# The opening of a fused attention and two-expert-layer kernel: first loads, first mask, sink loads, order of transposes and evacuations

## The reference

```python
# q, k, v: (2, 8, 768, 64); n_sink = 4, window = 128
scores = scale * np.matmul(q, k.transpose(0, 1, 3, 2))
keep = is_sink | in_window                  # key < 4, or 0 <= query - key < 128
scores = np.where(keep, scores, -1e9)
a = softmax(scores)
x = (a @ v) as (1536, 512)                  # heads side by side

h = x @ w_in                                # (512, 2048)
y = (max(h, 0) + alpha * min(h, 0)) @ w_out # (2048, 512)

e = argmax(y @ w_gate)                      # 8 experts, 384 places each
out = gate * (max(y @ w1[e], 0) @ w2[e])    # (512, 1024), (1024, 512)
```

## Time and profile before

| | us |
|---|---|
| median of 3 runs | 615.85 |
| lowest and highest | 614.84, 617.77 |
| the profiled execution | 616.75 |
| its span in the profile | 615.0 |
| PE busy in the span | 594.3 |
| PE's first matmul of scores | 6.5 |
| first matmul of `hidden(0)` | 41.18 |

### The profile page before, as it was taken

The page is one execution under the profiler, slowest core; times in us unless marked ns, Lnnn a source line. Parts: engine busy times, 40 slices in busy tenths (PEclk is TensorE's granted clock), DMA queues, the critical chain, the costliest instruction groups (busy, mean ns, idle before and its releaser), DMA issues.

```text
span 615.0 us, 11559 instructions
## 1 busy us (share of the span) xinstructions
PE 594.3 (97%) x3917; PEld 506.5 (82%) x3917; DVE 354.0 (58%) x1035; ACT 281.7 (46%) x681; POOL 144.5 (23%) x186
## 2 busy tenths in 40 slices
PE   8899999999999999999999999998999999999994
PEld 7677888888888888888888899988888888878883
DVE  4578876565556555665556445454754578489300
ACT  5676554433343334433433221122755588589320
POOL 5222222212112222122122100003302143245201
PEclk9899999999999999999999999997999999999998
DMA  7435440201052302010000060016672869499000
GB/s 174 138 86 155 139 139 18 70 18 37 19 172 70 86 17 70 19 35 18 36 1 18 2 206 0 1 43 215 244 253 70 292 226 376 155 353 347 31 19 19
DMA packets 73239, 67.45 MB, mean 110 GB/s; under 512 B 42852, under 2 KB 49012, under 8 KB 73168
## 3 DMA queue, kind: packets, MB, share of 16 engines
q1 hardware_dynamic: 69488, 57.76, 29.8%
q0 software_dynamic: 3680, 8.77, 4.5%
HBM read 57.75 MB, written 12.06 MB: 113 GB/s over the span
## 4 chain that ended last, share of the span: by engine, by line
PE 85%; DMA 4%; DVE 3%; ACT 3%; issue 2%; SPq 1%; POOL 0%; ACTq 0%; DVEq 0%; POOLq 0%
PE bank L960 22%; PE bank L962 21%; PE bank L961 21%; PE bank L950 10%; PE bank L1032 4%; PE bank L1004 4%; PE bank L1100 1%; DMA fw<-in_moe_w_dram 1%; ACT wh L705 1%; DMA fw<-y_scratch,mask 1%; DMA o_sb<-in_k_dram 1%; DMA o_sb<-in_q_dram 1%; DVE wl L1309 1%; DVE rw L1330 1%; PE bank L1047 1%
## 5 line engine op out<-in xcount | busy, mean ns | idle before, releaser
L960 PE MATMUL bank<-wh,rw 128*128 128x512 f32 x416 | 167.3, 402 | 1.9 <-DVE rw L1519 1.3
L962 PE MATMUL bank<-wh,rw 128*128 128x512 f32 x416 | 163.2, 392 | 0.0
L961 PE MATMUL bank<-wl,rw 128*128 128x512 f32 x416 | 162.9, 391 | 0.0
L960 PE MATMUL bank<-rw,wh 128*128 128x256 f32 x384 | 112.7, 293 | 0.0
L962 PE MATMUL bank<-rw,wl 128*128 128x256 f32 x384 | 108.3, 282 | 0.0
L961 PE MATMUL bank<-rw,wh 128*128 128x256 f32 x384 | 108.1, 282 | 0.0
L837 ACT CAST rw<-fw 128x256 fp32r<-128x256 f32 x96 | 39.0, 406 | 143.5 <-DVE fw L1513 143.1
L962 PEld LDWEIGHTS bank<-wh,rw 128*128 128x128 f32 x416 | 78.1, 188 | 17.1
L623 POOL TENSOR_SCALAR fw<-fw,rinv 128x256 f32<-128x256 f32 (+1 forms) x88 | 76.0, 874 | 68.4 <-DVE rinv L1364 68.2
L960 PEld LDWEIGHTS bank<-wh,rw 128*128 128x128 f32 x416 | 78.5, 189 | 16.0 <-DVE rw L1519 1.9
L961 PEld LDWEIGHTS bank<-wl,rw 128*128 128x128 f32 x416 | 78.5, 189 | 12.5
(11 more groups left out here) (118 smaller groups left out, 675.5 us busy)
## 6 DMA issues: line engine op xcount, KB each, us to landing
fw<-in_moe_w_dram SPq DMA_DIRECT2D x95, 256.0 KB, 5.4
v_raw<-in_moe_w_dram SPq DMA_DIRECT2D x22, 256.0 KB, 5.6
fw<-in_moe_w_in_dram SPq DMA_DIRECT2D x16, 256.0 KB, 3.4
fw<-in_moe_w_out_dram SPq DMA_DIRECT2D x16, 256.0 KB, 2.8
o_sb<-in_q_dram SPq DMA_DIRECT2D x12, 256.0 KB, 3.3
o_sb<-in_k_dram SPq DMA_DIRECT2D x12, 256.0 KB, 3.8
y_scratch<-fw SPq DMA_DIRECT2D x12, 256.0 KB, 2.1
out_dram<-v_or_route SPq DMA_DIRECT2D x12, 256.0 KB, 3.5
```

Source lines behind the costliest of these rows:

```text
L960: pe.matmul(dst, ah, bh, start=start, stop=False, skip_group_check=True)
L961: pe.matmul(dst, ah, bl, start=False, stop=False, skip_group_check=True)
L962: return pe.matmul(dst, al, bh, start=False, stop=stop, skip_group_check=True)
```

## The change

- **First loads.** q of tile 0 comes in two loads on SP (the first pair's two heads, then the other six), k of tile 0 in two loads on ACT's own queue. ACT issues them before anything else. The first pair has semaphores of its own.
- **First transposes.** PE transposes the first pair of q, does one filler, transposes the first pair of k, and then the rest of both; pair 0 of q is not transposed a second time.
- **Constants.** POOL makes the mask of tile 0 directly behind the identity; DVE waits for 5 constants in step 0 and for all 17 in step 1.
- **Low part of q.** The second part of tile 0's q is subtracted before `mask_max(0)` rather than behind it.
- **Sinks.** The 24 loads of the first batch go two a step in steps 8 to 19.
- **Transposes of q and k of tiles 1 and 2** move from steps 5 and 13, ahead of the scores, to steps 6 and 14, behind the scores, in the place of five fillers.
- **Step 22** keeps the opening's order: scores before values, `inverse` before `mask_max`, exponential before `evac_p`. Fillers stay out of it.
- **`split_by`.** No piece in step 2 any more, so one piece fewer by step 21, and another pattern from step 22 on. By the end of each step it gives:

| step | 22 | 23 | 26 | 29 | 30 | 31 | 32 | 33 | 34 | 35 | 36 | 37 |
|---|---|---|---|---|---|---|---|---|---|---|---|---|
| before | 10 | 12 | 17 | 22 | 23 | 25 | 27 | 28 | 30 | 32 | 32 | 32 |
| after | 9 | 11 | 15 | 21 | 22 | 24 | 25 | 27 | 28 | 30 | 31 | 32 |

```diff
 def split_by(n):
-    early = sum(k % 2 == 0 and k % H != 0 for k in range(min(n + 1, OPEN)))
-    late = sum(1 + (k % 3 != 0) for k in range(OPEN, n + 1))
+    early = sum(k > 2 and k % 2 == 0 and k % H != 0 for k in range(min(n + 1, OPEN)))
+    late = sum(1 + (k % 2 == 1 or k in (OPEN, OPEN + 6)) for k in range(OPEN, n + 1))
...
# SP
-            load_q(0)
-            load_k(0)
+            sp.dma_start(heads(q_raw)[:, 0:2, :], rows_of(q, 0)[:, 0:2, :]).then_inc(first_q_loaded, 16)
+            sp.dma_start(heads(q_raw)[:, 2:H, :], rows_of(q, 0)[:, 2:H, :]).then_inc(q_loaded, 16)
             load_v(0)
...
-                if n == 2:
-                    load_sinks(0)
+                if H <= n < H + 12:
+                    load_sinks(0, 2 * (n - H), 2 * (n - H) + 2)
...
# POOL
+            made(pool.memset(mask[:, 0, :], 0.0))
+            c = mask[:, 0, 0:P]
+            made(pool.affine_select(out=c, in_=c, compare_op=ALU.is_ge, fill=NEG,
+                                    base=0, pattern=[[-1, P]], channel_multiplier=1))
+            made(pool.memset(mask[:, 0, 0:n_sink], 0.0))
+            assert done[0] == NFIRST, done
             made(pool.memset(ones[:, :], 1.0))
...
# ACT
+            act.dma_start(heads(k_raw)[:, 0:2, :], rows_of(k, 0)[:, 0:2, :]).then_inc(first_k_loaded, 16)
+            act.dma_start(heads(k_raw)[:, 2:H, :], rows_of(k, 0)[:, 2:H, :]).then_inc(k_loaded, 16)
             qk_high(0, 0)
...
-                if n >= OPEN and moved is not None:
+                if n > OPEN and moved is not None:
                     evac_p(moved)
...
-                if n < OPEN and moved is not None:
+                if n <= OPEN and moved is not None:
                     evac_p(moved)
...
# PE
             keep_busy(10, Y_BANK[1])
-            first_pair_T(q_loaded, O_BANK, q_raw)
+            first_pair_T(first_q_loaded, O_BANK, q_raw)
+            keep_busy(1, Y_BANK[1])
+            first_pair_T(first_k_loaded, P_BANK, k_raw)
             q_T(0)
-            keep_busy(3, Y_BANK[1])
-            first_pair_T(k_loaded, P_BANK, k_raw)
             k_T(0)
             keep_busy(3, Y_BANK[1])
...
-                t = tile_at(n, -3)
-                if t is not None and early(t):
-                    q_T(t)
-                    k_T(t)
...
-                opening = n < OPEN
+                opening = n <= OPEN
...
-                filling = opening and n % 2 == 0 and n != TPC * H
+                filling = n < OPEN and n % 2 == 0 and n != TPC * H
...
                     scores(p, c, i)
-                if filling:
+                t = tile_at(n, -2)
+                if t is not None and early(t):
+                    q_T(t)
+                    k_T(t)
+                elif filling:
                     keep_busy(5, unread)
...
# DVE
                 if n == 0:
-                    dve.wait_ge(constants_made, NCONST)
+                    q_low(0, 1)
+                if n < 2:
+                    dve.wait_ge(constants_made, NCONST if n else NFIRST)
                 ended = pair_at(n, 2)
-                if n < OPEN and ended is not None:
+                if n <= OPEN and ended is not None:
                     inverse(ended)
```

More of the change, by code:

```diff
@@ L203, in sparse_attention_then_two_expert_layers @@
         output_zeroed = sem("output_zeroed")
+        first_q_loaded = sem("first_q_loaded")
+        first_k_loaded = sem("first_k_loaded")
         q_loaded = sem("q_loaded")
@@ L274, in sparse_attention_then_two_expert_layers @@
         last_yT_evacuated = sem("last_yT_evacuated")
-        NCONST = 15
+        NFIRST, NCONST = 5, 17
         RS = 26
@@ L427, in each_step, with rows_of, heads @@
                     step(c, i, H * TPC * (c + 1) + i + AHEAD)
+        def rows_of(x, t):
+            return x[t // QT, :, t % QT * P:(t % QT + 1) * P, :].rearrange("h p d -> p h d")
+        def heads(tile):
+            return tile.rearrange("p (h d) -> p h d", h=H)
         def pair_at(n, lag):
@@ L449, in load_piece @@
                 sp.dma_start(dst, src).then_inc(loaded, 16)
-            def rows_of(x, t):
-                return x[t // QT, :, t % QT * P:(t % QT + 1) * P, :].rearrange("h p d -> p h d")
-            def heads(tile):
-                return tile.rearrange("p (h d) -> p h d", h=H)
             def load_q(t):
-                if t:
-                    sp.wait_ge(q_transposed, t)
+                sp.wait_ge(q_transposed, t)
                 sp.dma_start(heads(q_raw), rows_of(q, t)).then_inc(q_loaded, 16)
             def load_k(t):
-                if t:
-                    sp.wait_ge(k_transposed, t)
+                sp.wait_ge(k_transposed, t)
                 sp.dma_start(heads(k_raw), rows_of(k, t)).then_inc(k_loaded, 16)
@@ L473, in load_v, with load_sinks @@
                 sp.dma_start(dst, rows_of(v, t)).then_inc(loaded, 16)
-            def load_sinks(b):
+            def load_sinks(b, lo, hi):
                 if b == 0:
@@ L479, in load_sinks @@
                     sp.wait_ge(v_sink_low_split, b)
-                for part in range(3):
-                    for h in range(H):
-                        r = (part * H + h) * n_sink
-                        sp.dma_start(v_sink[r:r + n_sink, h // 2, DH * (h % 2):DH * (h % 2) + DH],
-                                     v[b, h, 0:n_sink, :]).then_inc(v_sink_loaded, 16)
-            load_q(0)
-            load_k(0)
+                for x in range(lo, hi):
+                    h, r = x % H, x * n_sink
+                    sp.dma_start(v_sink[r:r + n_sink, h // 2, DH * (h % 2):DH * (h % 2) + DH],
+                                 v[b, h, 0:n_sink, :]).then_inc(v_sink_loaded, 16)
+            sp.dma_start(heads(q_raw)[:, 0:2, :], rows_of(q, 0)[:, 0:2, :]).then_inc(first_q_loaded, 16)
+            sp.dma_start(heads(q_raw)[:, 2:H, :], rows_of(q, 0)[:, 2:H, :]).then_inc(q_loaded, 16)
             load_v(0)
@@ L509, in step @@
                 if n % (H * QT) == 3 and H * QT < n < NH:
-                    load_sinks(n // (H * QT))
+                    load_sinks(n // (H * QT), 0, 3 * H)
                 if c >= 1 and i == 0:
@@ L594, in _ @@
                            allow_small_or_imprecise_dtypes=True))
-            made(pool.memset(mask[:, :, :], 0.0))
-            for m, s in [(0, 0), (1, 1), (2, 0), (3, 1)]:
+            made(pool.memset(mask[:, 1:4, :], 0.0))
+            for m, s in [(1, 1), (2, 0), (3, 1)]:
                 c = mask[:, m, s * P:(s + 1) * P]
@@ L606, in _ @@
                                         base=window - P, pattern=[[1, P]], channel_multiplier=-1))
-            made(pool.memset(mask[:, 0:2, 0:n_sink], 0.0))
+            made(pool.memset(mask[:, 1, 0:n_sink], 0.0))
             assert done[0] == NCONST, done
@@ L969, in q_T @@
                     pe.wait_ge(qk_low_split[1][0], t)
-                for r in range(PPT):
+                for r in range(t == 0, PPT):
                     x = tr(q_bank(t)[:, r * P:(r + 1) * P], q_raw[:, r * P:(r + 1) * P])
@@ L1492, in head_step @@
                 if t is not None and t < OPENING:
-                    q_low(t, 1)
+                    if t:
+                        q_low(t, 1)
                     k_low(t, 1)
-                if n >= OPEN and ended is not None:
+                if n > OPEN and ended is not None:
                     inverse(ended)
```

## The result

The changed kernel takes **624.14 us** (median of 6 runs, 621.57 to 629.57) against 616.41 us (6 runs, 614.70 to 620.21) for the kernel before beside it: ratio 1.0129, 95% interval 1.0079 to 1.0179. It is slower, by 1.3%. The forecast was 622.4, with the range 617.6 to 626.0. Ratios and intervals in this document are taken from executions in the chip's usual, fast state alone, so they aren't exactly the quotients of the medians beside them.

A forecast was written before the change was run, and what follows sets the result against it. PE bounds the kernel, busy 97% of the span. Opening 5.0 us won, table stalls 8.3 and clock 3.3 lost: 616.75 - 5.0 + 8.3 + 3.3 = 623.35, median 622.4, range 617.6 to 626.0.

The forecast's parts named there:

- The table: Steps 33 to 35: y_sum(10), (11) and (12) each wait 2.8 us for a piece, 8.3 us lost.
- the sum: Profiled time before, less the opening's gain, plus stalls and clock: 616.75 - 5.0 + 8.3 + 3.3 = 623.35, median 622.4.
- Met by the step before: All other y_sum of the sixteen have their pieces by the step before, so they were counted as no loss.
- The clock: Behind the three stalls PE's clock falls two times of three, at 1.65 us each: 3.3 us lost.
- The sinks: Opening: without 24 loads ahead of tile 2's q, its wait and the low clock go: 3.4 us won.
- Step 22: End of the opening: with scores and transposes ahead, hidden(0) starts right behind x's low part: 0.4 us won.
- Start and tile 1: Opening up to pair 6: earlier first scores and scores ahead of tile 1's transposes: 1.2 us won, start included.
- my 0.6: Start: first scores 0.6 us sooner, by smaller first loads, k's loads beside q's, and fewer fillers and transposes.
- contention only: Rival, start: two queues share the DMA engines, k comes as late as before; 0.6 off the gain; no chance given.

The follow-up runs named there:

- e1: The changed kernel with the old split_by table, all opening edits kept: 611.41 us, 0.9917 of before.
- e10: The changed kernel unaltered, timed again beside a version with filled waits: 623.95 us, 1.0148 of before.
- e2: The kernel before with the new split_by table alone: 628.10 us, 1.0198 of before.
- e9: e1 with one piece fewer at the end of step 33 only, so y_sum(11) alone waits: 616.56 us, 1.0013 of before.
- e5: The kernel before with only the first batch of sinks' loads spread two a step over steps 8 to 19: 611.72 us, 0.9942 of before.
- e7: e1 with step 22 back in its old order on PE, ACT and DVE: 610.62 us, 0.9936 of before.
- e8: e1 with four more fillers at the start, ahead of the rest of q's and k's transposes: 611.28 us, 0.9921 of before.
- e6: e1 with the old start (tile 0's q and k whole on SP, old order of transposes and fillers): 611.11 us, 0.9940 of before.
- e3: The changed kernel with one piece more in step 32 of the table: 612.02 us, 0.9971 of before.

## Why the prediction was right, point by point

**The table** was right in place, number and size: three waits of 2.81 us, 8.4 in all, where the sum had 8.4 less 0.1. Taken between starts of instructions a wait is a little dearer: from the last product of `hidden(m+1)` to `y_sum(m)` 83.36 - 80.27 = 3.09 us instead of 0.12, and the first product behind it takes 0.08 more, so 3.05 each; the small waits that were there before (0.28 and 0.06, and 0.08 behind each) came to 0.5. Three times 3.05 less 0.5 is 8.65. With the clock's 2.75 (383.07 - 380.32) it is 11.4; the table costs 11.8 (e1). The other 0.4 lies at two more places, seen when the starts of all blocks are laid beside e1's: 0.2 each at `y_sum(6)` and `y_sum(14)`. These need 18 and 31 pieces, and by the step before there are 19 and 31, one fewer than with the old table. DVE gets to the one that they need so late in that step that they start 0.17 us late. "Met by the step before", which the sum took as free, cost a little there.

**The clock** was right in count, two of three, and a little too dear: 3.3 in the sum, 2.75 measured. My 1.65 a fall came from the earlier trace rows, where PE went on with transposes and scores behind the wait for q; here a fall cost 1.2 and 1.5. The reason I gave was poorer than the result. "Two of three" was a middle between none and all, with an argument that stalls of 2.8 are like the waits of 1.9 and 2.5; that the count came out at two was luck. The first of them (in the changed kernel, in e10 and in e2), and e9's, had no such effect. A wait's length alone didn't decide it here.

**The sinks** were right: 3.4 expected, 3.4 measured (e5), by the wait and the low clock named. SP's rows in the changed kernel show what replaced the 8.27 us of the earlier trace rows: two loads ahead of q's, which is issued at 16.90 and no longer at 20.82.

```profile
16.17 0.69 SPq L482 DMA_DIRECT2D fw<-in_v_dram  x2
16.90 0.58 SPq L463 DMA_DIRECT2D o_sb<-in_q_dram  x1
```

**Step 22** was right at `hidden(0)` (0.4, e7), and 0.3 of it arrives.

**Start and tile 1** is the step that failed. It was to give 1.2 us, with 0.6 of it at the first scores. They came 0.6 later, at 7.16 (0.5 later by the means below). PE's timeline of the changed kernel:

```profile
1.59 2.39 PE L957 MATMUL bank<-ident 128*128 128x128 f32 x10 [1.59 <-POOL ident L584]
3.78 0.42 PE L957 MATMUL bank<-ident,o_sb 128*128 128x128 f32 x1
3.99 0.42 PE L957 MATMUL bank<-ident 128*128 128x128 f32 x1
4.21 0.42 PE L957 MATMUL bank<-ident,o_sb 128*128 128x128 f32 x1
4.83 1.76 PE L957 MATMUL bank<-ident,o_sb 128*128 128x128 f32 x7 [0.21 <-DMA o_sb<-in_q_dram]
6.38 0.85 PE L957 MATMUL bank<-ident 128*128 128x128 f32 x3
7.16 0.55 PE L1011 MATMUL bank<-rw 64*128 64x128 f32 x6
```

The first loads by their issues (queue, count, KB each, us from issue to landing):

```profile
o_sb<-in_q_dram SPq DMA_DIRECT2D x1, 192.0 KB, 3.5
o_sb<-in_k_dram ACTq DMA_DIRECT2D x1, 192.0 KB, 3.9
o_sb<-in_k_dram ACTq DMA_DIRECT2D x1, 64.0 KB, 2.3
o_sb<-in_q_dram SPq DMA_DIRECT2D x1, 64.0 KB, 2.1
```

Two things went wrong. The first is what stands ahead. The first pair of q, issued at 0.81, lands 2.1 us later at about 2.9, and that of k at about 3.1. But ten fillers stand ahead of their transposes, and PE, which begins them at 1.59, goes from them to q's transpose at 3.78 without a wait. In before the transposes had stood for all of q until 3.85 (0.26 us by the weight load ahead of them), so the split could win no more than 0.07 here. The rest of q, issued at 1.30, lands 3.5 us later at 4.8, and PE stands for it; k moved forward and q's rest back.

The second is the pace. All 13 transposes and fillers from 3.78 to the first scores are 0.21 to 0.22 us apart, where before those from 5.48 on stood 0.11 to 0.12 apart; that costs about 1 us (2.33 less 1.35, by e8), more than the products that went are worth. They are two fillers and one transpose: three fillers made way for one, and the prediction counted three gone. PE's wait for q's rest goes with the slow pace. In e7 there was no such wait, the transposes came closer together sooner, and the first scores stood at 6.15.

The section "Issuing engines are not separate DMA queues" of the Trainium skill, "DMA: Bandwidth & Descriptors", weighed in the prediction against my 0.6, fits this: with q's and k's rests issued side by side neither was quick (3.5 and 3.9 us). No run has the split without the second queue, so that this sharing is the cause is not shown. The last rival, contention only, was the nearest for this step: it took off the 0.6 hoped for at the first scores, and another 0.6 went beyond that. Its own condition, k as late as before, didn't hold: k's first transpose stands at 4.21, where before it stood at 5.48. What came late was q's rest.

And the start varies more than it did: over nine traces with the new start the first scores lie between 6.15 (e7, q's rest without a wait) and 7.70 (e9), mean 7.15; over four with the old start between 6.50 and 6.93, mean 6.66. Leave out e8 with its fillers, and they come the later the longer PE waited for q's rest: 6.15 without a wait, 6.97 and 7.16 with 0.2 us, 7.20 to 7.30 with 0.3, 7.54 with 0.6 and 7.70 with 0.75.

From the first scores on, the edits other than the sinks and step 22 win 1.7 - 0.4 = 1.3, more than the 0.6 that the sum kept for tile 1 alone. Start and tile 1 together come to 0.7 instead of 1.2, and the opening to 4.5 (`hidden(0)` at 36.66, forecast 36.2) instead of 5.0.

**The sum.** At the last logits it is -4.5 + 11.9 = +7.4, where the forecast had -5.0 + 8.3 + 3.3 = +6.6. Two misses of 0.5 and 0.3 went the same way. One gain that I didn't list came on top and went again: the gathers' wait was 1.3 us shorter than in the earlier trace rows, and 2.9 us of "issue" behind it took more than that back. No edit of the change touches that stage.

**The better kernel** is e1 or any of its kin: the new opening with the old table, 611.41 us, 0.9917 of before. e6, with the old start too, is at 611.11. Which of e1, e6, e7 and e8 is best the times don't tell. By the mean of the starts it would be e6: in its trace `hidden(0)` stands 5.0 us sooner than before (36.15 against 41.18) without the split loads.

## What to carry to other kernels

When a table says how much of some side work is done by when, count it against the need at every step, and look for the steps where it ends up one short. A surplus of none was nearly free here (28 of 28 in before; 0.6 us at most, in e3). One short costs the whole chain up to that piece (here 2.8 us, three times over), not the piece's 0.7 us. Small transfers in an in-order queue cost what they hold up, so spread them to where nothing waits behind. Before splitting a first load, look at what its reader does until then: here the first part was ready 0.9 us before PE got to it, since ten fillers stood ahead, and the rest came later than the whole load had.

## What the runs showed of the hardware

- A wait of PE of 2.81 us between stretches of full work left the granted clock at 1.00 (the first in the changed kernel, in e10 and in e2, and e9's only one). The second and third of a series, some 7.6 and 7.2 to 7.5 us behind the one before, were each followed by a window at 0.57 or 0.67, in after, e10 and e2. The wider spacing began 0.3 to 1.5 us after PE had gone on (after and e2). In before a single wait of 1.94 us in the opening, where PE was busy less, was followed by 0.50. Which property of the time before decides it, these runs don't settle; no run has two such waits further apart.
- The first transposes start 0.21 us apart and later 0.11 to 0.12, while the granted clock is shown as 1.00 all the time. The faster spacing came at about 5.0 us in before and 6.9 in after, where PE had a gap of 0.21 and fewer fillers: 6 products in one microsecond, then 11, both at 1.00. In e8, with more fillers, the transposes from 5.66 on stood closer already.

```profile
5.00:6.00 1.00, 1.00 (x6) 1.00 (x7) 0.25 (x1) 0.23 (x1) 0.67 (x3) 1.00 1.27 336
7.00:8.00 1.00, 1.00 (x11) 0.77 (x10) 0.14 (x1) 0.18 (x1) 0.18 (x2) 1.00 1.05 391
```

- The stretch behind the last logits took 199.9 to 205.9 us in the thirteen traces, though no edit touches it. That is 6 us, beside the 8 us over which the whole times of the changed kernel scatter (621.57 to 629.57).
